# Cluster marks of a masked attention made in lots of four heads, most of them amid the attention loop

## The chip, the core and the metric

The kernel runs on one core of a Trainium2 chip. A core has five engines that run side by side, each through its own instructions in order: PE (TensorE, matrix products), DVE (VectorE), ACT (ScalarE), POOL (GpSimd) and SP, which here only issues transfers. They signal one another through semaphores. The metric is the device time of one execution in microseconds, taken as the median of several.

## What is computed

Two batches of eight heads with 768 tokens of 64 values go through an attention in which a query sees only keys of its own cluster. The result goes through two feed-forward layers.

```
q_assign = argmax(einsum('bhsd,hcd->bhsc', q_n, c_n))      # 16 centroids for each head
k_assign = argmax(einsum('bhsd,hcd->bhsc', k_n, c_n))
mask = q_assign[..., :, None] == k_assign[..., None, :]
scores = where(mask, scale * q @ k.T, -1e9)
attn_out = softmax(scores) @ v                             # 2 x 8 heads x 768 x 64
x = attn_out as (1536, 512)
h = x @ moe_w_in;   x = (h * sigmoid(1.702 h)) @ moe_w_out      # inner width 2048
h = x @ moe2_w_in;  x = layernorm(h * softmax(h)) * g @ moe2_w_out   # inner width 1024
```

## The kernel before, in words

**Marks of clusters.** A query's cluster becomes a column of 16 rows with a 0 in the row of its cluster and 1 elsewhere, a key's a column with -2^100 in its row and 0 elsewhere. They are appended to q and k as rows 64 to 79 (`q_high`, `k_low`), so the product of scores adds the mask by itself. The marks are made in eight lots. In the kernel before, a lot is one of q or k, one batch (eight heads) and half of the tokens (384). Its steps: `load_pairs` (SP, four head pairs of 64+64 rows, 768 KB), `sims_of` (PE, four products with the centroids into 4 x 32 rows of a PSUM bank), `copy_sims` (ACT, to `sims_t`), `tokens_of` (PE, three transposes, L465), `compare` (DVE, L919 and L921: a maximum for each token and head, and where it is reached), `rank_lot` (POOL, L1244, for the first of equals), `choose` (DVE, L930 and L935), `hots_of` (PE, transposes back, L476, for two lots at once) and `store_clusters` (ACT, L715, to `hot_t`; the second batch, and later reads of the first, go through `mask_rows` in HBM). All eight `compare`s and six of eight `choose`s stand ahead of the attention loop, the rest in its first steps.

**Attention.** It runs over 8 iterations (`it`) of two heads each; an iteration has 12 steps (`n`), and a step handles 128 queries against 768 keys. Numbers are split into a high and a low part for accuracy (`k_high`, `k_low`, and so on). In one step:

- PE: `turn` (L519, six transposes of the probabilities of the step six before), `scores_of` (L502 and L506, four products), and a third of `head_half` (L534): the product with v of half a head (three steps), 12 matmuls cut by `HEAD_SPLIT`. In steps n with n mod 3 = 0 stand the first 3, with n mod 3 = 1 the next 5, and with n mod 3 = 2 the last 4. The last 4 stand ahead of the step's scores, the others behind them.
- DVE: `row_max` (L959), sums and inverses for two steps at once (L967, L973), `x_sum` (L986, every third step, frees the bank `head_out` for the next half head), `turned_low` (L979, twice).
- ACT: `turned_high` (L772, twice), `exps` (L761), every third step `x_of_low_v` (L778), and `kq_high` (L728) once for each head.
- POOL: `scale_q`, `kq_low` (L1158, the low part of a head's q and k), the scaling of the probabilities by their sums (L1221), splits of v.
- SP: `place_head` moves the parts of a head (64 rows to other 64 rows, L328), waits for them, and then places its 16 rows of marks (L336).

PE runs one step ahead of the others. Transposes use a ring of three PSUM banks (`pt_bank`). Iteration 0 is written out, the others are a loop (`Fori`) on every engine, in which semaphores are compared with registers.

**Behind the attention** follow the first layer (three blocks; its weights come in `gelu_turn` and are split by POOL) and the second layer. The second layer's weights are loaded 512 KB at a time by `load_ln`, once in each iteration.

## Time and profile before

| | us |
|---|---|
| time before, median of 3 runs | 671.55 (671.33 to 674.67) |
| the profiled execution | 672.1 |
| span in its trace | 670.3 |

The profile shows, for each engine, when each instruction ran and for what the engine had waited. A line of the timeline gives start, duration, engine, source line, operation, what it writes and reads, the shape, and how many like it were merged; in square brackets stand the idle time ahead of it and what ended it. The chain of waits goes back from the last instruction, at each step to what released it. Attention's first scores start at 31.5 us and its last step is over at about 250 us. The first layer runs to about 530 us.

### The profile page before, as it was taken

What the parts mean: (1) busy time and instruction counts of PE and PEld (TensorE: products, weight loads), DVE (VectorE), ACT (ScalarE), POOL (GpSimd) and SP (SyncE); (2) the same over time, 40 slices, a digit from 0 to 9 for tenths busy, and PEclk for the clock granted to TensorE, in tenths of its full rate; (3) what the DMA queues carried; (4) which work ended last, traced back from release to release, by engine and by line L of the source; (5) the groups of instructions that cost most, each with busy time, mean ns of one, the idle gap of its engine ahead of it and who ended that gap; (6) DMA issues with size and microseconds to landing.
All of it is one profiled execution on the core that took longest, in us unless ns stands there. A gap on an engine that the chain in (4) does not pass through costs nothing.

```text
span 670.3 us, 11572 instructions
## 1 busy us (share of the span) xinstructions
PE 639.0 (95%) x3281; PEld 537.8 (80%) x3281; DVE 434.5 (65%) x759; ACT 321.0 (48%) x641; POOL 419.7 (63%) x590
## 2 busy tenths in 40 slices
PE   5689999999999999999999999999999999999998
PEld 1369989898989888788877888788888878888886
DVE  3779999999999985666657667562222554545352
ACT  1279999999999984222232222132222243324232
POOL 2677788798888886888878888878886100000000
PEclk9779999999999999999999999999999999999999
DMA  8866544544544421232222222222231022112101
GB/s 284 245 185 154 159 120 112 143 122 126 143 112 137 130 92 64 72 113 87 104 94 93 90 99 94 94 95 94 94 106 51 29 82 77 52 60 78 63 16 47
DMA packets 39601, 70.52 MB, mean 105 GB/s; under 512 B 4256, under 2 KB 22688, under 8 KB 39584
## 3 DMA queue, kind: packets, MB, share of 16 engines
q1 hardware_dynamic: 37568, 66.38, 33.1%
q10 hardware_dynamic: 2016, 3.93, 1.6%
q8 instruction: 8, 0.13, 0.1%
q14 instruction: 9, 0.07, 0.0%
HBM read 46.60 MB, written 4.72 MB: 77 GB/s over the span
## 4 chain that ended last, share of the span: by engine, by line
PE 68%; ACT 10%; issue 9%; DVE 5%; DMA 4%; POOL 2%; DVEq 1%; SPq 1%; ACTq 0%; POOLq 0%
PE banks L534 6%; PE banks L549 6%; PE banks L551 6%; PE banks L550 6%; PE banks L564 6%; PE banks L566 6%; PE banks L565 5%; PE banks L639 5%; ACT probs L761 4%; PE banks L519 4%; PE banks L672 3%; PE banks L671 3%; PE banks L670 3%; ACT probs_th L772 3%; PE banks L642 2%
## 5 line engine op out<-in xcount | busy, mean ns | idle before, releaser
L979 DVE TENSOR_TENSOR probs_tl<-banks,probs_th 128x384 fp32r<-128x384 f32 x192 | 100.5, 547 | 11.7 <-ACT probs_th L772 9.4
L959 DVE TENSOR_REDUCE neg_max<-banks 128x1 f32<-128x768 f32 x96 | 91.3, 951 | 8.6 <-PE banks L506 6.6
L772 ACT CAST probs_th<-banks 128x384 fp32r<-128x384 f32 x192 | 83.0, 485 | 20.8 <-PE banks L519 19.5
L761 ACT ACTIVATE probs<-banks,neg_max 128x768 f32<-128x768 f32 x96 | 88.3, 920 | 7.1 <-DVE neg_max L959 7.0
L953 DVE TENSOR_TENSOR gl<-gate,gh 128x512 fp32r<-128x512 f32 x48 | 48.2, 1003 | 66.8 <-ACT gh L746 66.8
L1145 POOL TENSOR_TENSOR wait_scrap<-half_power 128x1 f32<-128x1 f32 x176 | 46.4, 264 | 67.1 <-PE banks L566 33.7
L1221 POOL TENSOR_SCALAR probs<-probs,row_inv 128x768 f32<-128x768 f32 x96 | 87.0, 907 | 0.0
L1284 POOL TENSOR_TENSOR stat<-stat,half_power 128x1 f32<-128x1 f32 x12 | 6.6, 549 | 127.5 <-DVE stat L1092 127.5
L519 PE MATMUL banks<-ident,probs 128*128 128x128 f32 x576 | 79.0, 273 | 1.3 <-ACT hot_t L715 1.3
L534 PE MATMUL banks<-probs_th,v_parts 128*128 128x384 f32 x192 | 70.4, 367 | 9.8 <-DVE x_sums L986 9.8
L746 ACT CAST gh<-gate 128x512 fp32r<-128x512 f32 x48 | 29.8, 621 | 101.1 <-PE banks L566 52.7
L549 PE MATMUL banks<-xh,uph 128*128 (+1 forms) x192 | 76.0, 396 | 0.4 <-POOL upl L1194 0.4
L564 PE MATMUL banks<-gh,downh 128*128 128x512 f32 x192 | 75.8, 395 | 0.2
L566 PE MATMUL banks<-gh,downl 128*128 128x512 f32 x192 | 75.3, 392 | 0.0
L551 PE MATMUL banks<-xh,upl 128*128 (+1 forms) x192 | 75.3, 392 | 0.0
L550 PE MATMUL banks<-xl,uph 128*128 (+1 forms) x192 | 75.1, 391 | 0.0
L565 PE MATMUL banks<-gl,downh 128*128 128x512 f32 x192 | 74.8, 390 | 0.0
L1204 POOL TENSOR_TENSOR downl<-gelu_raw,downh 128x512 fp32r<-128x512 f32 x48 | 71.4, 1488 | 4.0
L519 PEld LDWEIGHTS banks<-ident,probs 128*128 128x128 f32 x576 | 68.5, 140 | 5.7 <-ACT hot_t L715 1.6
L742 ACT ACTIVATE gate<-banks 128x512 f32<-128x512 f32 x48 | 28.7, 599 | 81.8 <-PE banks L551 57.0
L1194 POOL TENSOR_TENSOR upl<-gelu_raw,uph 128x512 fp32r<-128x512 f32 x48 | 62.7, 1306 | 4.0
L534 PE MATMUL banks<-probs_tl,v_parts 128*128 128x384 f32 x192 | 65.1, 339 | 0.0
(100 smaller groups left out, 1346.1 us busy)
## 6 DMA issues: line engine op xcount, KB each, us to landing
gelu_raw<-w_gelu SPq DMA_DIRECT2D x48, 512.0 KB, 3.3
ln_raw<-w_ln SPq DMA_DIRECT2D x8, 512.0 KB, 4.3
pair_t<-q_t SPq DMA_DIRECT2D x4, 768.0 KB, 7.3
pair_t<-k_t SPq DMA_DIRECT2D x4, 768.0 KB, 8.2
kq_raw<-k_t SPq DMA_DIRECT2D x16, 192.0 KB, 3.5
kq_raw<-q_t SPq DMA_DIRECT2D x16, 192.0 KB, 3.7
q_parts<-k_high SPq DMA_DIRECT2D x16, 192.0 KB, 2.6
q_high<-k_high SPq DMA_DIRECT2D x16, 192.0 KB, 3.0
```

What stands on the lines that cost most here:

```text
L519: last = nc.tensor.transpose(pt_bank(n, c)[:, t * P:(t + 1) * P], probs[:, n % NP, k * P:(k + 1) * P], ident[:])
L534: last = nc.tensor.matmul(head_out, v_parts[j][:, i // 2].rearrange("p two d -> p (two d)"), part[half % 2][:, i // 2, :], start=i == 0, s ...
L549: nc.tensor.matmul(hidden[u], uph[u][:, cols], xh[:, k, tok], start=k == 0, stop=False)
L550: nc.tensor.matmul(hidden[u], uph[u][:, cols], xl[:, k, tok], start=False, stop=False)
L551: last = nc.tensor.matmul(hidden[u], upl[u][:, cols], xh[:, k, tok], start=False, stop=k == KT - 1)
L564: nc.tensor.matmul(acc[d], downh[u][:, cols], gh[u][:], start=first, stop=False)
L565: nc.tensor.matmul(acc[d], downh[u][:, cols], gl[u][:], start=False, stop=False)
L566: last = nc.tensor.matmul(acc[d], downl[u][:, cols], gh[u][:], start=False, stop=end)
L761: nc.scalar.activation(probs[:, n % NP, :].rearrange("p (c t) -> p c t", c=2), scores[n % 2], ACT.Exp, bias=neg_max[:, n % NP:n % NP + 1], ...
L772: nc.scalar.copy(probs_th[half % 2][:, c * CH:(c + 1) * CH, i * P:(i + 1) * P], pt_bank(n, c).rearrange("p (t s) -> p t s", t=CH)).then_in ...
L959: nc.vector.tensor_reduce(out=neg_max[:, col], in_=scores[n % 2], op=ALU.max, axis=mybir.AxisListType.XY, negate=True).then_inc(max_done, 1)
L979: nc.vector.tensor_tensor(probs_tl[half % 2][at], pt_bank(n, c).rearrange("p (t s) -> p t s", t=CH), probs_th[half % 2][at].bitcast(F32), ...
```

## The change

- A lot is now q **and** k of four heads (a quad) for half of the tokens, eight rows of 16 each side by side: rows 0 to 63 of `hot_t` are the marks for q, rows 64 to 127 those for k, and the factor of `store_clusters` is a vector (`mask_scale`). So lots 0 and 1 serve iterations 0 and 1, lots 2 and 3 iterations 2 and 3, and so on. `choose` writes its tile in two halves, one for q and one for k.
- Only lots 0 and 1 stand ahead of attention. Lot e of the others starts in step 1 (even e) or 7 (odd e) of iteration 0, 2 or 4: `sims_of` and `copy_sims` in that step, `rank_lot` one step on in POOL's order, `tokens_of` and `compare` two steps on, `choose` five, `hots_of` and `store_clusters` seven.
- The lots share the ring of three banks with the transposes: `unit_of` numbers all uses in PE's order, and `take_bank` waits until the use three before is over.
- `mask_rows` is gone: `place_head` copies the marks from `hot_t` by a transfer within SBUF. SP loads quad 0, the q and k of heads 0 and 1, places head 0, and then loads quad 1.
- `HEAD_SPLIT` becomes (0, 4, 8, 12), and all three thirds stand behind the scores of their step.
- The loop over iterations is written out on all engines, with constants in the waits.
- `load_ln` is called four times in each of the last two iterations.

```diff
...
-        KQ_STEP, STORE_STEPS, HOT_STEPS, CHOOSE_STEPS = 0, (2, 4), (3, 5), (0, 1)
+        KQ_STEP = 0
+        EARLY_LOTS = 2
+        LOT_STARTS = (1, 7)
+        SIMS_AT, RANK_AT, CHOOSE_AT, HOT_AT = 2, 1, 5, 7
+        def lot_start(e):
+            return (e // 2 - 1) * 2 * STEPS + LOT_STARTS[e % 2]
+        def lots_at(it, n, offset):
+            return [e for e in range(EARLY_LOTS, LOTS) if lot_start(e) + offset == it * STEPS + n]
+        unit_of = {}
+        for what in ("sims_t", "sims", "hot"):
+            for e in range(EARLY_LOTS):
+                unit_of[what, e] = len(unit_of)
+        for g in range(ITS * STEPS + TURN_LAG + AHEAD):
+            if g >= TURN_LAG + AHEAD:
+                for c in range(2):
+                    unit_of["turn", g - TURN_LAG - AHEAD, c] = len(unit_of)
+            for what, offset in (("sims_t", 0), ("sims", SIMS_AT), ("hot", HOT_AT)):
+                for e in lots_at(0, g, offset):
+                    unit_of[what, e] = len(unit_of)
...
+        def bank_free(unit):
+            if unit < TURN_BANKS:
+                return []
+            what, *which = unit_names[unit - TURN_BANKS]
+            if what == "turn":
+                return [(pt_low_done, 2 * which[0] + which[1] + 1)]
+            return [({"sims_t": sims_t_copied, "sims": compared, "hot": hot_t_done}[what], which[0] + 1)]
...
-                b, x, c = e // 4, e // 2 % 2, e % 2
-                if b > 0:
-                    sp.wait_ge(sims_t_done, e - 3)
-                half = slice(c * HALF, (c + 1) * HALF)
-                sp.dma_start(pair_t[x][:, :, half], (q_pairs, k_pairs)[x][b][:, :, half]
-                             ).then_inc(pair_loaded[x][c], 16)
+            def load_pairs(quad):
+                b, at = quad // 2, slice(quad % 2 * 2, quad % 2 * 2 + 2)
+                if quad >= 2:
+                    sp.wait_ge(sims_t_done, (quad - 1) * 2)
+                for c in range(2):
+                    half = slice(c * HALF, (c + 1) * HALF)
+                    for x in range(2):
+                        sp.dma_start(pair_t[x][:, at, half], (q_pairs, k_pairs)[x][b][:, at, half]
+                                     ).then_inc(pair_loaded[c], 16)
...
-                    src = mask_heads[x, bass.ds(h, 1)].rearrange("o c s -> (o c) s")
-                    if isinstance(it, int) and it == 0 and j == 0:
-                        sp.wait_ge(hot_t_done, x + 1)
-                        src = hot_t[x][0:C, :]
-                    sp.dma_start(dst.bitcast(F32), src).then_inc(qk_ready[j], 16)
+                    at = x * QUAD * C + h % QUAD * C
+                    sp.dma_start(dst.bitcast(F32), hot_t[h // QUAD % 2][at:at + C, :]).then_inc(qk_ready[j], 16)
...
-            for e in range(4):
-                load_pairs(e)
-            load_kq(0, 0)
-            for e in range(4, LOTS - 1):
-                load_pairs(e)
-            load_kq(0, 1)
+            load_pairs(0)
+            sp.dma_start(gains_sb[:], gains).then_inc(gains_loaded, 16)
+            for j in range(2):
+                load_kq(0, j)
             place_head(0, 0)
-            for x in range(2):
-                sp.wait_ge(hot_t_done, x + 1)
-                sp.dma_start(mask_rows[x, 0], hot_t[x][:]).then_inc(mask_stored[x], 16)
-            for j in range(2):
-                load_v(0, j)
+            load_pairs(1)
+            load_v(0, 0)
             load_kq(1, 0)
-            for x in range(2):
-                sp.wait_ge(mask_stored[x], 16)
             place_head(0, 1)
...
+            for it in range(1, ITS):
                 load_kq(it, 1)
                 place_head(it, 0)
                 load_v(it, 0)
-                if not last:
+                if it < ITS - 1:
...
+                if it % 2 == 1 and it // 2 + 2 < NQUAD:
+                    load_pairs(it // 2 + 2)
+                if it >= ITS - 2:
+                    sp.wait_ge(sims_done, LOTS)
+                    for part in range((it - ITS + 2) * ITS // 2, (it - ITS + 3) * ITS // 2):
+                        load_ln(part)
+            for j in range(2):
+                sp.wait_ge(qk_ready[j], 48 * ITS)
...
             def sims_of(e):
-                b, x, c = e // 4, e // 2 % 2, e % 2
-                pe.wait_ge(pair_loaded[x][c], (b + 1) * 16)
-                if e >= 4:
-                    pe.wait_ge(sims_t_copied, e - 3)
-                for n in range(HP):
-                    last = nc.tensor.matmul(sims_t_ps[x][n * 2 * C:(n + 1) * 2 * C, c, :], c_diag[:, n, :],
-                                            pair_t[x][:, n, c * HALF:(c + 1) * HALF], start=True, stop=True)
+                quad, c = e // 2, e % 2
+                pe.wait_ge(pair_loaded[c], (quad + 1) * 32)
+                dst = take_bank("sims_t", e)
+                for n in range(4):
+                    x, pair = n // 2, quad % 2 * 2 + n % 2
+                    last = nc.tensor.matmul(dst[n * 2 * C:(n + 1) * 2 * C, :], c_diag[:, pair, :],
+                                            pair_t[x][:, pair, c * HALF:(c + 1) * HALF], start=True, stop=True)
                 last.then_inc(sims_t_done, 1)
...
-                x, c = e // 2 % 2, e % 2
                 pe.wait_ge(sims_t_copied, e + 1)
-                if e >= 2:
-                    pe.wait_ge(compared, e - 1)
+                dst = take_bank("sims", e)
                 for i in range(CH):
-                    t = c * CH + i
-                    last = nc.tensor.transpose(sims[c][:, i * P:(i + 1) * P], sims_t[x][:, t * P:(t + 1) * P],
+                    last = nc.tensor.transpose(dst[:, i * P:(i + 1) * P], sims_t[e % 2][:, i * P:(i + 1) * P], ident[:])
+                last.then_inc(sims_done, 1)
...
+            def hots_of(e):
+                pe.wait_ge(hot_done, (e + 1) * 2)
+                dst = take_bank("hot", e)
+                for i in range(CH):
+                    last = nc.tensor.transpose(dst[:, i * P:(i + 1) * P], hot[e % RANKS][:, i * P:(i + 1) * P],
                                                ident[:])
-                last.then_inc(sims_done, 1)
...
-            for e in range(4):
-                sims_of(e)
-                if e >= 1:
-                    tokens_of(e - 1)
-            for e in range(4, LOTS):
-                tokens_of(e - 1)
-                sims_of(e)
-                if e < 6:
-                    hots_of(e - 4)
-            tokens_of(LOTS - 1)
+            for of in (sims_of, tokens_of, hots_of):
+                for e in range(EARLY_LOTS):
+                    of(e)
...
-                    if exists(it, n, 2 - c, STEPS):
-                        pe.wait_ge(pt_low_done, 2 * g - 2 + c)
+                    dst = take_bank("turn", g, c)
...
-            HEAD_SPLIT = (0, 3, 8, 12)
+            HEAD_SPLIT = (0, 4, 8, 12)
...
             def attention_turn(it, steps=STEPS, drain=False):
                 for n in range(steps):
-                    first = isinstance(it, int) and it == 0
-                    if first and n in HOT_STEPS:
-                        hots_of(2 + HOT_STEPS.index(n))
-                    if first and n == TURN_LAG + AHEAD:
-                        pe.wait_ge(hot_t_done, LOTS // 2)
                     if exists(it, n, TURN_LAG + AHEAD, STEPS) and not (drain and n >= TURN_LAG + AHEAD):
                         turn(*lagged(it, n, TURN_LAG + AHEAD, STEPS))
-                    for c, lag in enumerate(HEAD_LAG + AHEAD + c for c in range(3)):
-                        if c in (2,) and exists(it, n, lag, STEPS) and (n - lag) % CH == CH - 1 and not (
-                                drain and n >= lag):
-                            head_half(*lagged(it, n, lag, STEPS), c)
                     if not drain:
                         scores_of(it, n)
                     for c, lag in enumerate(HEAD_LAG + AHEAD + c for c in range(3)):
-                        if c in (0, 1) and exists(it, n, lag, STEPS) and (n - lag) % CH == CH - 1 and not (
+                        if exists(it, n, lag, STEPS) and (n - lag) % CH == CH - 1 and not (
                                 drain and n >= lag):
                             head_half(*lagged(it, n, lag, STEPS), c)
+                    for of, offset in ((sims_of, 0), (tokens_of, SIMS_AT), (hots_of, HOT_AT)):
+                        for e in lots_at(it, n, offset):
+                            of(e)
...
+                if e >= 2:
+                    act.wait_ge(sims_done, e - 1)
+                nc.scalar.copy(sims_t[e % 2][:], turn_bank(unit_of["sims_t", e])).then_inc(sims_t_copied, 1)
+            def store_clusters(e):
+                quad, c = e // 2, e % 2
+                act.wait_ge(hot_ps_done, e + 1)
+                if e == 0:
+                    act.wait_ge(mask_scale_set, 2)
+                if quad >= 2:
+                    for j in range(2):
+                        act.wait_ge(qk_ready[j], 48 * 2 * (quad - 1))
+                nc.scalar.activation(hot_t[quad % 2][:, c * HALF:(c + 1) * HALF], turn_bank(unit_of["hot", e]), ACT.Copy,
+                                     scale=mask_scale[:]).then_inc(hot_t_done, 1)
...
-                if g >= 2:
-                    dve.wait_ge(hot_ps_done, g - 1)
-                nc.vector.tensor_tensor(heads(hot[x][:, c * HALF:(c + 1) * HALF]), ranks,
-                                        most[:].unsqueeze(2).to_broadcast([P, G, C]),
-                                        ALU.is_equal if x else ALU.not_equal).then_inc(hot_done, 1)
-            for b in range(B):
-                for e in range(4 + CHOICE_LAG):
-                    if e < 4:
-                        compare(b * 4 + e)
-                    if e >= CHOICE_LAG and b * 4 + e - CHOICE_LAG < LOTS - len(CHOOSE_STEPS):
-                        choose(b * 4 + e - CHOICE_LAG)
+                if e >= RANKS:
+                    dve.wait_ge(hot_ps_done, e - RANKS + 1)
+                for x in range(2):
+                    def side(ap):
+                        return ap.rearrange("p (i x h c) -> p i x h c", i=CH, x=2, c=C)[:, :, x]
+                    most = rank_max[r][:].rearrange("p (i x h) -> p i x h", i=CH, x=2)[:, :, x]
+                    nc.vector.tensor_tensor(side(hot[r][:]), side(rank[r][:]),
+                                            most.unsqueeze(3).to_broadcast([P, CH, QUAD, C]),
+                                            ALU.is_equal if x else ALU.not_equal).then_inc(hot_done, 1)
...
-            for e in range(LOTS):
+            scale_q(0, 0)
+            for e in range(EARLY_LOTS):
                 rank_lot(e)
-                if e == 2:
-                    scale_q(0, 0)
-                if e == 3:
-                    for c in range(2):
-                        kq_low(0, 0, c)
-                if e == 4:
-                    scale_q(0, 1)
+            for c in range(2):
+                kq_low(0, 0, c)
+            scale_q(0, 1)
             for c in range(2):
...
```

PE ahead of attention. `pair_t` holds q and k as loaded, `sims_t` the copied products, `hot` the marks by token. In the kernel before, the eight rows before the first scores, and the scores:

```order
L465 MATMUL banks<-ident,sims_t 128x128 x3
L453 MATMUL banks<-pair_t,c_diag 32x384 x4
L476 MATMUL banks<-ident,hot 128x128 x6
L465 MATMUL banks<-ident,sims_t 128x128 x3
L453 MATMUL banks<-pair_t,c_diag 32x384 x4
L465 MATMUL banks<-ident,sims_t 128x128 x3
L453 MATMUL banks<-pair_t,c_diag 32x384 x4
L465 MATMUL banks<-ident,sims_t 128x128 x3
L502 MATMUL banks<-k_high,q_parts 128x384 x2
```

In the changed kernel, from the products of both early lots on:

```order
L481 MATMUL banks<-pair_t,c_diag 32x384 x8
L489 MATMUL banks<-ident,sims_t 128x128 x6
L497 MATMUL banks<-ident,hot 128x128 x6
L516 MATMUL banks<-k_high,q_parts 128x384 x2
L520 MATMUL banks<-k_low,q_high 128x384 x2
L516 MATMUL banks<-k_high,q_parts 128x384 x2
L520 MATMUL banks<-k_low,q_high 128x384 x2
L481 MATMUL banks<-pair_t,c_diag 32x384 x4
```

Two lots are left ahead of the scores, and the third one's products (last row) follow behind the scores of step 1.

PE within attention, a step with n mod 3 = 2 (`probs_th`, `probs_tl` are the turned probabilities of a half head). Before:

```order
L512 REGISTER_ALU
L516 ISA
L519 MATMUL banks<-ident,probs 128x128 x3
L516 REGISTER_ALU
L519 MATMUL banks<-ident,probs 128x128 x3
L534 MATMUL banks<-probs_th1,v_parts0 128x384
L534 MATMUL banks<-probs_tl1,v_parts0 128x384
L534 MATMUL banks<-probs_th1,v_parts0 128x384
L534 MATMUL banks<-probs_tl1,v_parts0 128x384
L498 REGISTER_ALU
L502 MATMUL banks<-k_high0,q_parts0 128x384 x2
L506 MATMUL banks<-k_low0,q_high0 128x384 x2
```

Changed, the same step of iteration 2, which also holds the products of no lot:

```order
L531 MATMUL banks<-ident,probs 128x128 x6
L516 MATMUL banks<-k_high0,q_parts0 128x384 x2
L520 MATMUL banks<-k_low0,q_high0 128x384 x2
L546 MATMUL banks<-probs_th1,v_parts0 128x384
L546 MATMUL banks<-probs_tl1,v_parts0 128x384
L546 MATMUL banks<-probs_th1,v_parts0 128x384
L546 MATMUL banks<-probs_tl1,v_parts0 128x384
```

The scores stand ahead of the last third of the half head, and the register instructions are gone.

DVE within attention, steps 2 and 3. Before (loop body):

```order
L959 TENSOR_REDUCE neg_max<-banks 128x1
L967 TENSOR_REDUCE row_sum_e<-row_sum 128x2
L984 ISA
L986 ISA x2
L986 TENSOR_TENSOR x_sums<-banks,x_sums 64x384
L977 ISA
L979 TENSOR_TENSOR probs_tl1<-banks,probs_th1 128x3x128
L973 RECIPROCAL row_inv<-row_sum_e 128x2
```

Changed, iteration 2, steps 5 and 6, where the choice of lot 4 stands:

```order
L994 TENSOR_TENSOR x_sums<-banks,x_sums 64x384
L986 TENSOR_TENSOR probs_tl0<-banks,probs_th0 128x3x128 x2
L966 TENSOR_REDUCE neg_max<-banks 128x1
L974 TENSOR_REDUCE row_sum_e<-row_sum 128x2
L986 TENSOR_TENSOR probs_tl0<-banks,probs_th0 128x3x128
L980 RECIPROCAL row_inv<-row_sum_e 128x2
L986 TENSOR_TENSOR probs_tl0<-banks,probs_th0 128x3x128
L933 TENSOR_REDUCE rank_max0<-rank0 128x24
L944 TENSOR_TENSOR hot0<-rank0,rank_max0 128x3x64 x2
L966 TENSOR_REDUCE neg_max<-banks 128x1
```

Three instructions of the lot stand between the low parts of step 6 and the row maxima of step 7; the register instructions between row maxima and `x_sums` are gone.

## Rows read from the trace of the kernel before

**Rows 1.** Timeline: PE ahead of attention (start us, duration us, engine, line)
```profile
9.75 0.90 PE L465 MATMUL banks<-ident,sims_t 128*128 128x128 f32 x3
```
**Rows 2.** Timeline: POOL ahead of attention
```profile
20.26 2.59 POOL L1158 TENSOR_TENSOR k_low<-kq_raw,k_high 128x384 fp32r<-128x384 f32 x2
```
**Rows 3.** Chain of waits, 20 to 60 us (start us, us, what)
```profile
22.87 5.32 DMA q_parts<-k_low
...
28.83 2.62 DMA k_low<-hot_t
...
43.08 0.71 ACT hot_t L715
43.81 4.06 DMA mask_rows<-hot_t
```
**Rows 4.** The page's transfers (count, size, median us to landing)
```profile
q_parts<-k_low SPq DMA_DIRECT2D x16, 192.0 KB, 2.7
```
**Rows 5.** Timeline: DVE, row maxima of iteration 0, steps 0, 5, 6, 7, 8
```profile
33.26 0.96 DVE L959 TENSOR_REDUCE neg_max<-banks 128x1 f32<-128x768 f32 x1 [1.37 <-PE banks L506]
...
42.58 0.96 DVE L959 TENSOR_REDUCE neg_max<-banks 128x1 f32<-128x768 f32 x1 [0.26 <-PE banks L506]
...
46.73 0.96 DVE L959 TENSOR_REDUCE neg_max<-banks 128x1 f32<-128x768 f32 x1 [0.77 <-PE banks L506]
...
48.65 0.95 DVE L959 TENSOR_REDUCE neg_max<-banks 128x1 f32<-128x768 f32 x1
...
50.44 0.95 DVE L959 TENSOR_REDUCE neg_max<-banks 128x1 f32<-128x768 f32 x1
```
**Rows 6.** Windows: stretch us, busy us of PE, PEld, DVE, ACT, POOL, PEclk, DMA share, GB/s
```profile
36.00:40.00 4.00, 4.00 (x15) 3.48 (x15) 2.99 (x7) 2.62 (x5) 3.61 (x6) 0.50 0.64 140
...
72.50:126.50 54.00, 51.25 (x337) 47.85 (x335) 50.57 (x105) 49.73 (x113) 45.53 (x68) 1.00 0.49 129
```
**Rows 7.** Waits, 72 to 234 us (in total, times, longest)
```profile
PE banks L534 <- DVE x_sums L986: 8.0, 25, 0.6
```
**Rows 8.** Timeline: one turn of three steps in iteration 4, all engines
```profile
136.79 0.92 ACT L761 ACTIVATE probs<-banks,neg_max 128x768 f32<-128x768 f32 x1
...
137.22 0.51 PE L506 MATMUL banks<-k_low,q_high 80*128 80x384 f32 x2
...
137.77 0.96 DVE L959 TENSOR_REDUCE neg_max<-banks 128x1 f32<-128x768 f32 x1
137.83 0.48 ACT L778 COPY x_sums<-banks 64x384 f32 x1
...
138.85 0.55 DVE L986 TENSOR_TENSOR x_sums<-banks,x_sums 64x384 f32 x1
...
139.46 0.45 PE L534 MATMUL banks<-probs_th,v_parts 128*128 128x384 f32 x1 [0.37 <-DVE x_sums L986]
```
**Rows 9.** Timeline: DVE in iteration 0, step 11, which has constants in its waits
```profile
56.51 0.96 DVE L959 TENSOR_REDUCE neg_max<-banks 128x1 f32<-128x768 f32 x1
57.38 0.54 DVE L986 TENSOR_TENSOR x_sums<-banks,x_sums 64x384 f32<-64x384 f32 x1
```
**Rows 10.** Timeline: the parts of a lot ahead of attention
```profile
24.35 0.85 PE L453 MATMUL banks<-pair_t,c_diag 128*32 128x384 f32 x8
24.46 0.56 DVE L919 TENSOR_REDUCE sims_max<-banks 128x24 f32<-128x384 f32 x1 [1.41 <-PE banks L465]
25.05 0.56 DVE L921 TENSOR_TENSOR rank<-banks,sims_max 128x384 f32<-128x384 f32 x1
...
25.53 0.54 DVE L930 TENSOR_REDUCE rank_max<-rank 128x24 f32<-128x384 f32 x1
25.70 1.00 POOL L1244 TENSOR_TENSOR rank<-rank,first_rank 128x384 f32<-128x384 f32 x1 [0.54 <-DVE rank L921]
...
26.11 1.00 DVE L935 TENSOR_TENSOR hot<-rank,rank_max 128x384 f32<-128x384 f32 x1
...
34.71 0.56 DVE L935 TENSOR_TENSOR hot<-rank,rank_max 128x384 f32<-128x384 f32 x1
```

148 lines of the change are left out of this document (63 added, 85 removed).

## Prediction

> **What bounds the kernel now.** I read the shares of the windows first, then who waits for whom, then the timeline of one turn of the attention loop, and last the chain of waits at the start. The change touches only the time up to the end of attention, about 250 of 670 us; the two layers behind it keep their work and order. Within attention no engine stands out: in 54 us, two iterations, PE is busy for 51.25, DVE for 50.57, ACT for 49.73 and POOL for 45.53 [rows 6]. So the loop goes round a chain through several engines. The waits name its seam: PE waits for DVE's `x_sum`, 25 times in 162 us for 8.0 us, so 0.33 us in every turn of three steps (about 6.75 us) [rows 7]. The timeline shows the turn: `exps` on ACT from 136.79, the copy of the half head from 137.83, `x_sum` on DVE at 138.85, and at 139.46 PE starts the next half head, behind which stand the transposes that ACT waits for next [rows 8]. `x_sum` starts 0.54 us after the copy is over (138.31) since DVE's row maxima hold it up, and they had waited until 137.73 for scores that stand behind the last third of the half head. The next most tightly loaded part is DVE: where it has no waits, a step goes by in 1.79 us (48.65 to 50.44, step 7 of iteration 0 [rows 5]); with the sums (about 0.13 in every second step) and an `x_sum` (0.5 in every third), three steps need some 6.1 of the 6.75 us. That leaves 0.6 us a turn, and this is where the lots go.
>
> **First term, the start: -8.9 us.** Now the first scores start at 31.45, at the landing of head 0's marks (28.83 + 2.62) [rows 3]. What the change leaves ahead of them: the first lot's load has the size of the first transfer before (768 KB), the second's as well, so PE turns the first lot's tokens at 9.75 as before [rows 1]. A lot's comparison takes 0.56 + 0.56 and two gaps of 0.03, so 1.2 us [rows 10]: over at 11.9 for lot 0 and 13.1 for lot 1, as the tokens of lot 1 follow at once, without a further lot's products between. POOL's ranking (1.00 [rows 10]) of lot 1 is over at 14.1, and then `kq_low` follows with 2.59 [rows 2], until 16.7; before, it was over at 22.85. The marks (choice, transposes, `store_clusters`) are ready at about 17.5, before they are asked for. The move of the low parts took 5.32 us here [rows 3] amid five other loads; the median of its 16 is 2.7 [rows 4]. Ahead of it now only head 1's 192 KB pieces are under way, so I take 2.8, with 5.3 as the other end: landed at 19.6. From there to the first scores it was 3.3 us before (28.19 to 31.45) [rows 3], and the transfers are the same. First scores at 22.6 instead of 31.5: -8.9, between -6.4 and -9.3.
>
> **Second term, the filling of the loop: -2.2 us.** In iteration 0 the row maxima of step 6 follow those of step 5 after 4.15 us (42.58 to 46.73), the next after 1.92 [rows 5]. In that gap ACT writes `hot_t` until 43.79 and `mask_rows` goes to HBM until 47.87 [rows 3]; PE waits for both. The change has neither at this place: -2.2. The clock stays as it was: it stood at 0.50, 1.2 GHz, from 36 to 40 us, nine microseconds into dense work, and at 1.00 later [rows 6], and I expect the same number of slow steps. Lot 2's products and tokens (twice 0.85 and 0.55 at the low clock) and its comparison fall into steps 1 to 3, where there are no transposes and half heads yet, and PE waits for `exps` of two steps ago: nothing. Head 1 must be placed until step 6, 13 us after the start; SP comes to it behind head 0, four loads of pairs, v and two more, some 5 us, then needs about 9 us as before (`kq_high` to landed marks). This is close; its bound is +2 us.
>
> **Third term, the turn of the loop: -7.2 us.** With the scores ahead of the last third, the row maxima before `x_sum` start when DVE is free, 0.1 us earlier in one kind of turn and 0.2 in the other. The constants in the waits take away two register instructions between them: in iteration 0, which has constants, `x_sum` starts 0.87 us after the row maxima [rows 9], in the loop 1.08 after (137.77 to 138.85) [rows 8]. In the turn shown this is 0.28, in the other kind 0.20, on average 0.24 us. It is less than PE's 0.33 of waiting, so PE doesn't take it back, and `HEAD_SPLIT` moves one matmul from the second to the first third, with the same sum ahead of the transposes. 30 turns by 0.24: -7.2. The bounds are -9.9 (all of PE's waiting) and 0, if ACT's copy now waits for the last third: by my count of PE's instructions that is over within 0.1 us of when ACT comes to it.
>
> **Fourth term, six lots amid attention: +15.2 us.** PE: 0.85 (products at the full clock) and twice 0.3 (transposes: 0.55 with the last one's run-out) [rows 10]. The products stand between the second third and the transposes that ACT waits for, so they count in full, 0.8. DVE: the comparison, 1.2 at the end of step 3 or 9; ahead of the next row maxima there is a slack of 0.4 (in the turn shown, ACT's `exps` start 0.4 us after their maxima), so it costs 0.8. The choice: a maximum of 0.54 and two halves of a tile that took 1.00 with POOL at work and 0.56 without (25.70 and 26.11 against 34.71) [rows 10]. The slow one ended at 27.11, 0.41 us after POOL's instruction (25.70 + 1.00). So I take it that a piece can't run beside POOL's reading of the same memory, and ends some 0.2 us behind POOL's current instruction, most of which take 0.9 to 1.0. The first half catches the rest of one of them, the second half a whole one: 0.55 + 0.35 + 1.1 = 2.0 us, less 0.4 of slack: 1.6. The ends are 0.7 (two halves of 0.28 and the maximum, less the slack) and 2.4. Marks turned back and stored fall where PE and ACT have 0.3 to 0.5 us to spare: nothing. The products of an odd lot stand one step behind an even lot's choice, in whose delay they disappear. So a pair of lots costs 0.8 + 0.8 + 1.6 + 0.8 + 1.6 = 5.6 us, and the first pair, whose first two items lie in the filling, 4.0: 15.2 in all. PE's work alone, 1.45 each, would give 8.7.
>
> The Trainium skill (SBUF — State Buffer, SBUF: two separate sides) states such a lock: a DVE instruction with two SBUF inputs and a GpSimd one exclude each other for a whole instruction. Without it, two halves at half of 1.00 would make the choice 1.55 us and this term about 12.5; the ends 0.41 us behind POOL's agree with the lock.
>
> **Nothing** for the rest: POOL has 8 of 54 us to spare for a ranking of 1.00; SP has fewer transfers; weights of the first layer start behind four more loads of 512 KB, some 5 us later, of which POOL's waits in the last iteration cover most (bound +1.5).
>
> **Sum.** 672.1 - 8.9 - 2.2 - 7.2 + 15.2 = 669.0 for an execution like the profiled one, which lies 0.55 above the median of the runs: 668.4.
>
> **The rivals.** (1) The lots vanish in the idle time of DVE and PE, down to PE's own 8.7: 662. For it speaks that a delay of DVE lets PE run ahead; against it, that the turn has 0.6 us of slack and a lot brings over 3 us. (2) Slower: DVE becomes the bound at the lots. If both halves of the choice wait for a whole instruction of POOL (2.8 us), and the ring of three banks, which a lot's use makes one narrower, lets PE wait for the low parts of the step just before, nothing of a lot is hidden: 1.2 + 2.8 on DVE and no slack, 4 us each, 24 in all: 677. It decides from 3.6 us a lot, where the sum passes 675. For it speaks DVE's load; against it, that iterations 1, 3, 5 to 7 are nearly free of lots. (3) The third term fails, as ACT waits for the half head: 675.5 by the sum. (4) The change doesn't start attention as early as it says, since head 0's moves or head 1's placement stay at their slow ends: 4 us less, 672.5.
>
> **Chances.** My sum 0.42, rival (1) 0.20, (2) 0.12, (3) 0.11, (4) 0.15. The range leaves out the far end of (2) and mixtures beyond (1): 661.5 to 676. A measurement of this kernel tells 0.5%, 3.4 us, from no change. Faster by more: all of (1) and half of my own case, whose middle lies 3.15 below: 0.42. Slower by more: (2) and two thirds of (3), 0.19. Within: the rest, 0.39.
>
> **What would show it.** In the trace of the changed kernel: first scores at 22.6 (right within 1 us); the row maxima of steps 5 to 7 of iteration 0 about 2 us apart; iterations 6 and 7, which have no lots, 26.0 instead of 27.0 us, with PE's waits for `x_sum` down to 0.1 a turn and `x_sum` 0.87 behind the row maxima; iterations 2 and 4 longer than those by about 4, and 3 and 5 by 1.6; halves of `hot` of about 0.35 and 1.1 us. A wrong third term shows as idle time of ACT ahead of the copy of the half head; a wrong fourth as waits of PE's transposes for low parts, or as lots without any trace in the cadence.

## The result, and the profile after

| | before | after |
|---|---|---|
| median, us (range, runs) | 673.11 (671.33 to 676.15, 4) | 693.34 (692.08 to 695.46, 4) |
| span of the profiled execution, us | 670.3 | 691.4 |

The ratio is 1.031 (95% interval 1.028 to 1.034): 3% slower, where 668.4 us and a range up to 676 were forecast.

A row maximum on DVE begins every step, so the distances of their starts are a ruler for attention. Iteration lengths (row maxima of step 0 to the next step 0), with two of the experiments (1 and 3) beside them:

| us | first row maxima | it 0 | 1 | 2 | 3 | 4 | 5 | 6 |
|---|---|---|---|---|---|---|---|---|
| before | 33.26 | 25.51 | 27.46 | 26.99 | 27.04 | 27.01 | 27.01 | 27.00 |
| after | 24.45 | 32.17 | 29.18 | 35.45 | 28.36 | 35.45 | 28.32 | 28.09 |
| without lots 2 to 7 | 23.71 | 24.56 | 26.21 | 26.18 | 26.20 | 26.21 | 26.23 | 29.52 |
| lots 12 steps apart | 25.70 | 27.89 | 32.39 | 32.39 | 32.39 | 32.38 | 32.39 | 26.65 |

Attention starts 8.8 us earlier, and a turn of the loop is shorter. Iterations 2 and 4 hold a whole even lot and the products and comparison of the odd one; they take 35.45 us instead of 27. Iterations 3 and 5 hold the odd lot's choice and marks and take 28.3. So a pair of lots adds 11.4 us to the 52.4 of two iterations without lots.

The chain of waits of the changed kernel at the start (answers [rows 3]; start us, us, what):

```profile
17.12 2.73 DMA q_parts<-k_low
...
20.48 2.16 DMA k_low<-hot_t
...
22.68 1.01 PE banks L516 x2
```

The low parts move in 2.73 us (5.32 before) and the first scores start at 22.68 us instead of 31.50.

The filling (answers [rows 5]): the timeline of DVE, row maxima of steps 5 and 6 of iteration 0, then PE's scores of step 6 and SP's moves of head 1:

```profile
33.90 0.94 DVE L966 TENSOR_REDUCE neg_max<-banks 128x1 f32<-128x768 f32 x1
38.73 0.96 DVE L966 TENSOR_REDUCE neg_max<-banks 128x1 f32<-128x768 f32 x1 [2.56 <-PE banks L520]
```

```profile
37.05 1.01 PE L516 MATMUL banks<-k_high,q_parts 128*128 128x384 f32 x2 [2.55 <-DMA k_low<-hot_t]
```

```profile
27.71 0.60 SPq L365 DMA_DIRECT2D q_high<-k_high  x1
29.22 0.46 SPq L365 DMA_DIRECT2D q_parts<-k_low  x1
33.27 0.46 SPq L365 DMA_DIRECT2D k_high<-k_high  x1
```

The step from 5 to 6 is 4.83 us, longer than the 4.15 that were to become 1.95: PE waits 2.55 us for head 1's marks. SP could issue `k_high`'s move at 33.27 only, since the move issued at 27.71 took 5.54 us to land. The loads of the second quad had been issued ahead of it; no run takes them away, so that they are the reason is argued.

PE's waits in the same gap of the kernel before (timeline of PE, iteration 0):

```profile
43.83 0.87 PE L519 MATMUL banks<-ident,probs 128*128 128x128 f32 x6 [1.29 <-ACT hot_t L715]
...
45.71 0.62 PE L502 MATMUL banks<-k_high,q_parts 128*128 128x384 f32 x2 [1.01 <-DMA k_low<-mask_rows]
```

There PE waited 1.29 us for ACT's marks and 1.01 us for the landing of head 1's rows of marks. It did not wait for the transfer to `mask_rows` until 47.87 [rows 3], as the row maxima of step 6 start at 46.73.

One turn of three steps in iteration 6, which has no lots (answers [rows 8]; timeline, ACT, DVE and PE):

```profile
197.84 0.95 DVE L966 TENSOR_REDUCE neg_max<-banks 128x1 f32<-128x768 f32 x1
...
198.11 0.47 ACT L780 COPY x_sums<-banks 64x384 f32<-64x384 f32 x1
...
198.82 0.56 DVE L994 TENSOR_TENSOR x_sums<-banks,x_sums 64x384 f32<-64x384 f32 x1
...
199.53 0.41 PE L546 MATMUL banks<-probs_th,v_parts 128*128 128x384 f32 x1
```

From the row maxima to `x_sum` it is 0.98 us (1.08 before, [rows 8]), and PE's half head has no wait ahead of it. Over the four turns of an iteration the distance is 0.86 to 1.04 us, 0.95 on average, against 1.02 before; the row maxima themselves start 0.27 us ahead of ACT's copy of the half head instead of 0.06. The windows of two iterations without lots, in the changed kernel without lots 2 to 7 (answers [rows 6]; stretch, us, busy us of PE, PEld, DVE, ACT, POOL, clock, DMA share, GB/s):

```profile
74.48:126.86 52.38, 51.29 (x338) 48.16 (x337) 50.22 (x105) 49.54 (x113) 45.76 (x69) 1.00 0.46 114
```

The same work as before, 1.6 us shorter, and PE busy for 98% of it.

Now the lots. The waits of PE in attention, 20 to 270 us (answers [rows 7]; in total, times, longest):

```profile
PE banks L516 <- DMA k_low<-hot_t: 9.0, 3, 4.2
PE banks L497 <- ACT sims_t L708: 7.0, 3, 2.4
PE banks L531 <- DVE rank L925: 5.2, 5, 1.1
PE banks L531 <- ACT sims_t L708: 2.4, 2, 1.2
PE banks L531 <- DVE probs_tl L986: 2.2, 3, 0.9
PE banks L489 <- ACT hot_t L720: 2.0, 3, 0.7
PE banks L546 <- DVE x_sums L994: 1.9, 7, 0.3
```

`x_sum`'s 8.0 us are down to 1.9. The first row is no wait on lots: it is the start, head 1 (2.55 us) and head 14 (2.29 us). The rows with `sims_t`, `rank` and `hot_t` are 16.6 us of new waits on lots. Iteration 2, the parts of lot 4 (PE products at L481, ACT's copy at L708, a turn at L531, comparison at L923 and L925, choice at L933 and L944):

```profile
88.00 0.85 PE L481 MATMUL banks<-pair_t,c_diag 128*32 128x384 f32 x8
...
91.65 0.48 ACT L708 COPY sims_t<-banks 128x384 f32<-128x384 f32 x1
...
92.27 0.85 PE L531 MATMUL banks<-ident,probs 128*128 128x128 f32 x6 [1.21 <-ACT sims_t L708]
...
96.66 0.55 DVE L923 TENSOR_REDUCE sims_max<-banks 128x24 f32<-128x384 f32 x1
...
97.24 0.56 DVE L925 TENSOR_TENSOR rank<-banks,sims_max 128x384 f32<-128x384 f32 x1
...
97.95 0.85 PE L531 MATMUL banks<-ident,probs 128*128 128x128 f32 x6 [1.05 <-DVE rank L925]
...
104.67 0.54 DVE L933 TENSOR_REDUCE rank_max<-rank 128x24 f32<-128x384 f32 x1
...
104.80 0.93 POOL L1235 TENSOR_SCALAR probs<-probs,row_inv 128x768 f32<-128x768 f32 x1
105.25 1.76 DVE L944 TENSOR_TENSOR hot<-rank,rank_max 128x192 f32<-128x192 f32 x2
...
105.66 1.14 POOL L1166 TENSOR_TENSOR k_low<-kq_raw,k_high 128x384 fp32r<-128x384 f32 x1
```

The products were over at 88.85, but ACT copied them at 91.65, since its copy stands at the end of a step, behind the exponentials; two steps on, the transposes that need the bank wait 1.21 us for it. The choice takes 0.54 + 1.76 = 2.3 us. The run with lots 12 steps apart shows one lot by itself. Its step lengths against those without a lot:

| step | what of the lot | without, us | with, us | more, us |
|---|---|---|---|---|
| 1 | products on PE | 1.80 | 2.63 | 0.83 |
| 2 | the turn waits for ACT's copy of them | 2.38 | 3.52 | 1.14 |
| 3 | tokens; comparison on DVE | 1.98 | 3.38 | 1.40 |
| 4 | | 2.12 | 2.30 | 0.18 |
| 6 | choice on DVE | 2.14 | 4.40 | 2.26 |
| 7 | | 2.00 | 1.80 | -0.20 |
| 9 | marks turned and stored | 1.87 | 2.44 | 0.57 |

These are 6.2 us for a lot by itself, all of it visible in the cadence. In the changed kernel a pair costs 11.4 and not 12.4: the odd lot's products in step 7 lengthen nothing (1.79 us against 1.80 with the even lot alone), as was forecast, and its choice costs 1.44 us (step 0 of iteration 3, 3.84 against 2.40).

Last, the layer norm's loads. SP in iterations 6 and 7 (timeline; then one row of the chain of waits, 222 to 245 us), and PE's scores of head 14 behind them:

```profile
222.40 1.98 SPq L388 DMA_DIRECT2D ln_raw<-w_ln  x4
...
230.51 0.46 SPq L365 DMA_DIRECT2D q_parts<-k_low  x1
236.94 0.46 SPq L365 DMA_DIRECT2D k_high<-k_high  x1
```

```profile
227.87 9.05 DMA q_high<-k_high
```

```profile
240.47 0.62 PE L516 MATMUL banks<-k_high,q_parts 128*128 128x384 f32 x2 [2.29 <-DMA k_low<-hot_t]
...
242.33 1.48 PE L531 MATMUL banks<-ident,probs 128*128 128x128 f32 x6
```

```profile
240.00:244.00 4.00, 3.54 (x16) 3.44 (x17) 1.30 (x3) 1.22 (x3) 1.98 (x3) 0.69 0.63 145
```

Behind four loads of 512 KB the move of head 14 issued at 227.87 lands after 9.05 us (the median of its 16 is 3.0), and SP issues `k_high`'s move 6.4 us after the one before it. PE waits 2.29 us. Its granted clock is then 0.69 on average over the four microseconds shown (0.50, 1.2 GHz, from 242 to 244 us), and six transposes take 1.48 us instead of 0.82.

### The profile page after: what moved, and what is told of

The parts are those of the page before. It is cut to its first block, busy times and chain, and to the rows that moved or that the text cites. A ratio compares the mean times of both kernels' runs of the same rounds, so it can differ in the third digit from the quotient of the medians.

```text
span 691.4 us, 10571 instructions
## 1 busy us (share of the span) xinstructions
PE 638.9 (92%) x3281; PEld 537.4 (78%) x3281; DVE 437.0 (63%) x769; ACT 322.0 (47%) x645; POOL 420.3 (61%) x590
## 4 chain that ended last, share of the span: by engine, by line
PE 63%; ACT 10%; DMA 8%; DVE 7%; issue 6%; POOL 5%; SPq 1%; DVEq 0%; POOLq 0%; ACTq 0%
PE banks L561 6%; PE banks L563 6%; PE banks L562 6%; PE banks L576 5%; PE banks L578 5%; PE banks L577 5%; PE banks L643 5%; PE banks L531 4%; PE banks L546 4%; ACT probs L762 4%; ACT probs_th L773 3%; PE banks L676 3%; PE banks L675 3%; PE banks L674 3%; PE banks L646 2%
## 5 line engine op out<-in xcount | busy, mean ns | idle before, releaser
L531 PE MATMUL banks<-ident,probs 128*128 128x128 f32 x576 | 80.8, 277 | 11.4 <-DVE rank L925 5.2
L531 PEld LDWEIGHTS banks<-ident,probs 128*128 128x128 f32 x576 | 68.1, 142 | 21.2 <-issue 12.2
L546 PE MATMUL banks<-probs_th,v_parts 128*128 128x384 f32 x192 | 67.4, 351 | 4.0 <-DVE x_sums L994 1.9
L516 PE MATMUL banks<-k_high,q_parts 128*128 128x384 f32 x192 | 59.5, 392 | 10.0 <-DMA k_low<-hot_t 9.0
```

What stands on the lines that cost most here:

```text
L531: last = nc.tensor.transpose(dst[:, t * P:(t + 1) * P], probs[:, n % NP, k * P:(k + 1) * P], ident[:])
L546: last = nc.tensor.matmul(head_out, v_parts[j][:, i // 2].rearrange("p two d -> p (two d)"), part[half % 2][:, i // 2, :], start=i == 0, s ...
```

## The experiments

Theory A: the lots cost more than they were priced at. Theory B: the start or the turn has failed and the lots are cheap. Within A three causes stood against each other: DVE's amount of work, the ring of three banks that a lot's use makes narrower, and order and locks at single places. Ratios are against the kernel before on the same chip.

### 1. Without lots 2 to 7 (`no_lots`)

```diff
-            return [e for e in range(EARLY_LOTS, LOTS) if lot_start(e) + offset == it * STEPS + n]
+            return []
-        LOTS = 2 * NQUAD
+        LOTS = 2
```

> The changed kernel without lots 2 to 7: their loads (but quad 1's), products, comparisons, rankings, choices, transposes and stores are left out, and all heads get the marks of quad 0. It measures what the six lots cost amid attention. Both theories: iterations 2 to 5 fall to 26.2 us each, the cadence that iteration 6 of the changed kernel shows, so 2 x 9.2 + 2 x 2.1 = 22.6 us less there, some 6 us less in iterations 0 and 1, and a time near 665. If iterations 2 to 5 stay over 27, the loop written out costs something by itself.

Measured: 660.34 us, ratio 0.982 (0.979 to 0.985); iterations of 26.2 us. So the lots cost 33 us, more than twice the 15.2 of the fourth term, and B falls. What is left is still 7 us above the 653.2 that the other terms give: iterations 6 and 7 are 3.3 and 1.6 us longer than in experiment 11, where the layer norm's loads are spread, and the filling is 1.2 and the turn some 1.2 us short of their terms.

### 2. Little work on DVE for these lots (`light`)

```diff
-                nc.vector.tensor_reduce(out=sims_max[r][:], in_=sim, op=ALU.max, axis=AX_X).then_inc(sims_max_done, 1)
+                nc.vector.tensor_reduce(out=sims_max[r][:, some], in_=sim[:, some], op=ALU.max, axis=AX_X).then_inc(sims_max_done, 1)
...
+                    if e >= EARLY_LOTS:
+                        nc.vector.tensor_tensor(side(hot[r][:])[:, 0, 0], side(rank[r][:])[:, 0, 0],
+                                                most[:, 0, 0:1].to_broadcast([P, C]),
+                                                ALU.is_equal if x else ALU.not_equal).then_inc(hot_done, 1)
+                        continue
```

(`some` is the first of 24 groups.)

> The changed kernel with DVE's work for lots 2 to 7 cut to one group of 16 columns of 24 (comparison, maximum and both halves of the choice: some 0.15 to 0.2 us each instead of 3.9 in all); PE, ACT, POOL and all waits stay. The marks of quads 1 to 3 are thus mostly left out. Theory of the ring (a lot's use of the three transpose banks ties PE to ACT's and DVE's current step, so that it loses its lead of one step): half or more of the 11.4 us a pair of lots stays, iterations 2 and 4 at 30 to 31 us. Rival, the work on DVE: iterations 2 and 4 fall to about 28 (26.2 and twice PE's 0.8), and PE's waits in the ring vanish with it.

Measured: 683.80 us, 1.017 (1.014 to 1.020). Nearly all of DVE's elements are gone, and 9.5 us with them; 23.5 are left. I read that at first as a proof against DVE and for the ring. It was neither, as experiments 4 and 8 show: step 6 still took 4.11 us, since the two tiny halves of the choice took 1.85.

### 3. Lots 12 steps apart (`apart`)

```diff
-        LOT_STARTS = (1, 7)
+        LOT_STARTS = (1, 13)
```

> The changed kernel with LOT_STARTS (1, 13) instead of (1, 7): the odd lot starts a whole iteration after the even one, with the same work. Then three uses ahead of the even lot's marks in the ring no longer stands the odd lot's product tile, on which PE waits 2.4 us for ACT's copy, nor the marks three ahead of the odd lot's tokens (0.7 us). Theory of the ring: 3 us less for each pair, 9 in all, a time of 684. Rival, the work on DVE: a lot more in one iteration and one less in the other, no change of the sum, 692 to 694.

Measured: 692.99 us, 1.031 (1.027 to 1.034), no change. The longest of the waits (2.4 us of a lot's marks for the next lot's copied products) is gone, and every lot costs 6.2 us by itself. A wait's length in the list was no price: others took its place.

### 4. Empty places in the ring (`empty_units`)

Experiment 1, but each lot's three places in the ring stay, unused:

```diff
-        LOTS = 2 * NQUAD
+        LOTS = 2
...
+        def lots_at(it, n, offset):
+            return []
...
-                for e in lots_at(0, g, offset):
+                for e in skipped_at(0, g, offset):
                     unit_of[what, e] = len(unit_of)
...
+            if what != "turn" and which[0] >= EARLY_LOTS:
+                return bank_free(unit - TURN_BANKS)
```

> The kernel without lots 2 to 7 (660.3 us), but every lot still takes its three places in the ring of three banks (products, tokens, hots; 18 places in all) and leaves them empty. No engine has work of these lots. So the time over 660.3 is the price of the narrower ring alone: after an empty place the second half of the next step's transposes must wait for the low parts of the step just before, and not of the one before that. With DVE's work of the lots nearly gone the time was 683.8, so PE's and ACT's work, the ring and the order share 23.5 us. PE's products and transposes are 1.45 us a lot, 8.7 in all. My theory, that most of the rest is the ring: 0.5 us a place, 669 us (666 to 673), with iterations 2 and 4 longest. Rival, the work itself in PE's and ACT's order is what costs, and a skipped bank by itself costs nothing: 660 to 662 us, all iterations at 26.2.

Measured: 662.44 us, 0.983 (0.979 to 0.987), and every iteration from 1 to 5 is 26.20 or 26.21 us. The windows of iterations 2 and 3, with the six empty places of a pair of lots:

```profile
77.24:129.65 52.41, 51.40 (x338) 48.12 (x337) 50.24 (x105) 49.61 (x113) 45.73 (x69) 1.00 0.47 114
```

The ring, the theory that I held after experiment 2, costs nothing in the loop by itself. (By the medians it is 2 us over experiment 1, but the traced execution, 659.59 us, is not longer than that of experiment 1, 660.57: iteration 0 is 2.05 us longer, where PE waits 2.3 us instead of 1.4 for head 1's marks, and iteration 6 is 2.2 shorter.) What costs is that a place is held until somebody has done its work.

### 5. The lots' pieces ahead of scores and exponentials (`copy_first`)

```diff
+                    for of, offset in ((sims_of, 0), (tokens_of, SIMS_AT), (hots_of, HOT_AT)):
+                        for e in lots_at(it, n, offset):
+                            of(e)
                     if not drain:
                         scores_of(it, n)
```

(PE; on ACT `copy_sims` and `store_clusters` go ahead of `exps` in the same way.)

> The changed kernel with the lots' pieces earlier within their step: on PE the products, tokens and hots go ahead of the scores instead of behind the half head's third, on ACT the copies of products and marks go ahead of the exponentials. Theory that the waits of PE's transposes for ACT's copy (1.2 us each, two in iterations 2 and 3) and for the marks' copy are what costs: they go, at about 1 us a lot, 687 us. Rival, by what the run with lots 12 steps apart showed: a delay around the ring only changes its name, since scores and row maxima now come 0.8 us later and DVE, with its comparison behind, has no slack: 690 to 697 us, with the waits of the copy gone and waits for DVE's low parts or comparison in their place.

Measured: 687.89 us, 1.019 (1.015 to 1.024): 5.4 us less by the medians, 7.7 by the ratios, each of which is known to 2 or 3 us. The theory had said 6. Step 2 is 0.33 us longer than without a lot instead of 1.14, iterations 2 and 3 are 33.8 and 27.7. A pair is 2.3 us cheaper, so the place of the pieces, on PE and ACT together, was about 1 us a lot. The rest stays.

### 6. The choice in one instruction (`one_choice`)

```diff
-                    nc.vector.tensor_tensor(side(hot[r][:]), side(rank[r][:]),
-                                            most.unsqueeze(3).to_broadcast([P, CH, QUAD, C]),
-                                            ALU.is_equal if x else ALU.not_equal).then_inc(hot_done, 1)
+                nc.vector.tensor_tensor(heads(hot[r][:]), heads(rank[r][:]),
+                                        rank_max[r][:].unsqueeze(2).to_broadcast([P, G, C]), ALU.is_equal
+                                        ).then_inc(hot_done, 2)
...
-                                     scale=mask_scale[:]).then_inc(hot_t_done, 1)
+                                     bias=mask_bias[:], scale=mask_scale[:]).then_inc(hot_t_done, 1)
```

> The changed kernel with the choice's two halves in one instruction (equal for q and k alike; the store of the marks turns q's side over by its scale and a bias). Same elements, one meeting with POOL's lock in the place of two: 1.76 + 0.54 us of choice should become about 1.0 + 0.54, the step that holds it 3.6 instead of 4.41 us, and the time 6 times 0.8 less: 688 us (686.5 to 690). Rival: DVE's wait at this place isn't the lock but the amount of work, and the number of instructions is indifferent: 693 us.

Measured: 687.72 us, 1.023 (1.020 to 1.026), 5 to 6 us less. Step 6 is 3.52 us instead of 4.41, with the same elements. (In iteration 2 the single instruction took 0.82 us, the two halves 1.76.) That the time came out as forecast is in part luck: 6 times 0.8 had been counted, but only the even lots gain. Iteration 2 is 0.8 us shorter and iteration 3 the same (28.32 against 28.36 us); of the rest in the trace, 2.55 us lie in iteration 0, where none was expected. Experiment 8 shows why the odd lots gain nothing.

### 7. One input in place of two (`light_one_input`)

Experiment 2 with another kind of tiny instruction:

```diff
-                        nc.vector.tensor_tensor(side(hot[r][:])[:, 0, 0], side(rank[r][:])[:, 0, 0],
-                                                most[:, 0, 0:1].to_broadcast([P, C]),
-                                                ALU.is_equal if x else ALU.not_equal).then_inc(hot_done, 1)
+                        nc.vector.tensor_scalar(side(hot[r][:])[:, 0, 0], side(rank[r][:])[:, 0, 0], 1.0, None,
+                                                ALU.mult).then_inc(hot_done, 1)
```

> The run with little work on DVE (683.8 us; of lots 2 to 7 one head in twelve times two is compared and chosen, and marked), and in addition each of the two small pieces that write the marks reads one tile of memory times 1.0 instead of comparing two tiles. In the 683.8 us run these two pieces of 16 columns still took 1.85 us, beside POOL's instructions, and the step that holds them was 4.11 us long where one without a lot takes 2.14. If that is the lock of DVE against POOL, and it needs two inputs in memory, the pieces fall to 0.2 us, the step to about 2.5 and the time by 6 times 1.5: 675 us (673 to 677). Rival: the pieces wait for something else that stands there (POOL's ranking, the transposes that read the tile), or one input is locked as well: 683.8 us.

Measured: 685.73 us, 1.021 (1.017 to 1.024); step 6 is 4.09 us, the pieces 1.85. My condition, two inputs, was wrong. It left open whether it is a lock at all.

### 8. A reduction in their place (`light_reduce`)

```diff
-                        nc.vector.tensor_tensor(side(hot[r][:])[:, 0, 0], side(rank[r][:])[:, 0, 0],
-                                                most[:, 0, 0:1].to_broadcast([P, C]),
-                                                ALU.is_equal if x else ALU.not_equal).then_inc(hot_done, 1)
+                        nc.vector.tensor_reduce(out=side(hot[r][:])[:, 0, 0, 0:1], in_=side(rank[r][:])[:, 0, 0],
+                                                op=ALU.max, axis=AX_X).then_inc(hot_done, 1)
```

> The run with little work on DVE (683.8 us), its two pieces at the place of the choice made a third kind of instruction: a tensor_reduce of 16 columns of the ranks into one column of the same tile (the marks are not chosen by it). If the 1.85 us are a lock against GpSimd that only some kinds of instruction meet, the pieces take 0.16 us each like the reduce ahead of them, the step falls from 4.11 to about 2.5 us (2.14 without a lot) and the time by 6 times 1.6: 674 us (672 to 677). If the wait belongs to the place or to the tile that is written, the step stays at 4.1 and the time at 684.

Measured: 679.42 us, 1.006 (1.004 to 1.009). By the ratios that is 7 us less than experiment 2 (by the medians 4.4; the kernel before was 2.4 us slower in this measurement), where 10 were expected. The trace is of an execution of 687.05 us, longer than the median; against the trace of experiment 2 it starts 1.3 us later and its iterations 0 and 6 are 3.2 and 2.9 us longer. The steps used here lie in iteration 2 at a clock of 1.00. The instructions themselves decide the question. First the timeline of DVE and POOL in experiment 2:

```profile
99.86 0.90 POOL L1243 TENSOR_SCALAR probs<-probs,row_inv 128x768 f32<-128x768 f32 x1
99.91 1.85 DVE L948 TENSOR_TENSOR hot<-rank,rank_max 128x16 f32<-128x16 f32 x2
100.73 1.00 POOL L1174 TENSOR_TENSOR k_low<-kq_raw,k_high 128x384 fp32r<-128x384 f32 x1
```

then the tiles `hot`, `rank_max` and `rank` in it (line, engine, operation, count: shortest/median/longest ns, first and last start):

```profile
L948 DVE TENSOR_TENSOR hot<-rank,rank_max x2: 874/962/1051, 99.9 to 100.7; 128x16 f32<-128x16 f32 x2
L936 DVE TENSOR_REDUCE rank_max<-rank x1: 160/160/160, 99.7 to 99.7; 128x1 f32<-128x16 f32 x1
L927 DVE TENSOR_TENSOR rank<-banks,sims_max x1: 174/174/174, 92.7 to 92.7; 128x16 f32<-128x16 f32 x1
```

the tile `hot` with one input:

```profile
L948 DVE TENSOR_SCALAR hot<-rank x2: 875/971/1067, 100.2 to 101.0; 128x16 f32<-128x16 f32 x2
```

and with reductions:

```profile
L948 DVE TENSOR_REDUCE hot<-rank x4: 158/166/172, 102.8 to 120.0; 128x1 f32<-128x16 f32 x4
```

Sixteen columns take 0.16 us by a reduction and 0.17 by a comparison one of whose inputs is a bank, but 0.87 and 1.05 by a comparison of two tiles and 0.88 and 1.07 by a product of one tile. In experiment 2 the first piece ends at 99.91 + 0.87 = 100.78, with POOL's instruction (99.86 + 0.90 = 100.76); the second at 101.76, with POOL's next (100.73 + 1.00 = 101.73). Two instructions in a row each wait for a whole instruction of POOL, whatever they have to do. The odd lot of the same run gives the other half of the comparison (timeline, then the tile `hot`):

```profile
118.32 1.01 POOL L1174 TENSOR_TENSOR k_low<-kq_raw,k_high 128x384 fp32r<-128x384 f32 x1
...
118.55 0.90 DVE L948 TENSOR_TENSOR hot<-rank,rank_max 128x16 f32<-128x16 f32 x2
```

```profile
L948 DVE TENSOR_TENSOR hot<-rank,rank_max x2: 163/490/816, 118.5 to 119.3; 128x16 f32<-128x16 f32 x2
```

The first piece ends at 118.55 + 0.82 = 119.37, with POOL's instruction (119.33). The second, the same instruction, takes 0.16 us: POOL has only an instruction of one column then. That is a lock against POOL, and it depends on the kind of instruction, as the comparison with an input in a bank (at 92.68) and the reductions (at 102.82) ran beside large instructions of POOL in 0.16 to 0.17 us. The choice met it twice in the even lots and once in the odd ones; in the changed kernel the two halves take 1.76 us in an even lot and 0.93 in an odd one. With reductions step 6 is 2.50 us instead of 4.11, 1.6 us less. But steps 7 and 8 grow by 0.65 and 0.13 (the end of one lot meets the start of the next), and a pair of lots gets cheaper by 2.2 us (62.28 to 60.06) and not by 3.2.

The Trainium skill (SBUF — State Buffer, Who interferes with whom) names both conditions: two SBUF inputs, or a kind of instruction that can use both ports, among them `tensor_scalar`; `tensor_reduce` never contends on this chip. The rows above agree.

### 9. PE alone (`pe_only`)

Experiment 7, with ACT's copies of products and marks cut from 384 to 8 columns.

```diff
-                nc.scalar.copy(sims_t[e % 2][:], turn_bank(unit_of["sims_t", e]))
+                cut = HALF if e < EARLY_LOTS else 8
+                nc.scalar.copy(sims_t[e % 2][:, 0:cut], turn_bank(unit_of["sims_t", e])[:, 0:cut])
```

> As the run with one input on DVE, and ACT's copies of products and marks of lots 2 to 7 cut from 384 to 8 columns (heads 4 to 15 get their marks' rows from the first four). PE's products, tokens and hots are all there: 1.45 us a lot, 8.7 in all. If PE has no slack and the other engines' parts are gone, 660.3 + 8.7 = 669 us (667 to 671), and the turn behind the products no longer waits 1.2 us for the copy, so ACT's part was the 5 to 6 us between. Rival: ACT's copies lie in its idle time and PE's place and order cost it all: no change against the run with one input (675).

Measured: 681.75 us, 1.014 (1.011 to 1.017), 4 us under experiment 7, not 6, and 21 over experiment 1. It is not PE alone: the tiny choice still meets the lock (step 6 4.09 us), and the turn in step 2 still waits 0.9 us for a copy of 8 columns, since the copy's place is late and not its length. Amounts of work on ACT explain 4 us.

### 10. Both taken away (`reduce_copy_first`)

Experiments 5 and 8 together.

> The same with the lots' pieces ahead of the scores on PE and ahead of the exponentials on ACT. Left of a lot are then PE's 1.45 us (8.7 in all over the 660.3 us without lots, so 669) and what ACT's two copies of 0.5 us push back. If waits behind ACT's place were most of the rest: 669 to 671 us, 4 below light_reduce. If it is only the amount of PE's and ACT's work that counts, their place changes nothing: 674.

Measured: 680.72 us, 1.009 (1.006 to 1.012), the same as experiment 8. Iterations 2 and 3 take 32.66 and 26.96 us, against 32.78 and 27.28. Its steps say why: step 2 is 0.8 us shorter and step 7 is 1.2 longer. In 75 to 135 us PE waits now at the lots' own transposes:

```profile
PE banks L489 <- ACT hot_t L720: 1.4, 1, 1.4
PE banks L497 <- ACT sims_t L708: 1.1, 1, 1.1
```

Moved ahead of the scores, marks and tokens of one lot come before ACT has emptied the bank of the other, and hold the scores up. So 7.2 us a pair stay (32.66 + 26.96 - 2 × 26.2), of which PE's own work is 2.9. The 4.3 between are not taken apart further.

### 11. The layer norm's loads spread (`ln_spread`)

```diff
+            PARTS = {(ITS - 3, 1): (0, 1), (ITS - 2, 0): (2,), (ITS - 2, 1): (3, 4), (ITS - 1, 0): (5,), (ITS - 1, 1): (6, 7)}
```

(one or two parts behind each head's v, instead of four at once)

> The changed kernel with the eight loads of the second layer's weights spread behind five placements of heads (2, 1, 2, 1, 2) instead of four each in the last two iterations. Theory of the loads: the move of head 14's low parts no longer lands 6.4 us after its issue, PE's 2.3 us wait at the start of iteration 7 and the slow clock behind it go, and the start of the first layer's weights comes earlier: 3 to 5 us less. Rival: the placement was late for another reason, no change.

Measured: 689.91 us, 1.026 (1.023 to 1.029), 3.4 us less; iteration 6 is 26.21 us instead of 28.09, and iteration 7 is 1.9 us shorter. Iterations 0, 2 and 4, which the edit doesn't touch, differ by -1.4, +0.9 and +0.9 us between the two traces, so single iterations with lots are known to about a microsecond only.

### 12. Three changes together (`all_three`)

Experiments 5, 6 and 11.

> Three changes on top of the changed kernel: the pieces of lots ahead of scores and exponentials (alone -5.4 us), the layer norm's loads spread over the last iterations (alone -3.4), and the choice in one instruction (expected -5). If they lie at different places they add up: 679.5 us (677.5 to 682). If the choice in one gives nothing: 684.5.

Measured: 684.43 us, 1.017 (1.013 to 1.020): 8.9 us less than the changed kernel, near 5.4 + 3.4, what experiments 5 and 11 gave by their medians (by the ratios it is 9 against 11, within the intervals). The choice in one gives nothing on top: step 6 is 3.50 us instead of 4.39, step 7 is 2.65 instead of 1.79. Again a gain at one place is given back at the next.

### 13. The kernel before with one part of the loop change, or both

`b_order`, the sums' thirds all behind the scores (the lines that ran the last third ahead of them go as well):

```diff
-            HEAD_SPLIT = (0, 3, 8, 12)
+            HEAD_SPLIT = (0, 4, 8, 12)
...
-                        if c in (0, 1) and exists(it, n, lag, STEPS)
+                        if exists(it, n, lag, STEPS)
```

> The kernel before with only one part of the change: HEAD_SPLIT (0, 4, 8, 12), and the last third of a half head behind the scores; loops stay. By the prediction's third term the row maxima start 0.1 to 0.2 us earlier in each turn: 0.6 us an iteration, 4.5 us less, 667. Rival: the gain comes only with constants in the waits, no change.

Measured: 674.09 us, 1.000 (0.998 to 1.002), iterations of 27.24 us. The waits of 90 to 144 us, two iterations, have two rows that the kernel before has not:

```profile
DVE x_sums L982 <- ACT x_sums L774: 2.2, 4, 0.6
...
ACT x_sums L774 <- PE banks L534: 1.2, 4, 0.3
```

With the new order alone ACT's copy waits for the last third in two of four turns, and `x_sum` for the copy, which is what the prediction named as the case in which its third term is 0.

`b_unroll`, the loops written out on all engines:

```diff
-            attention_turn(0)
-            with pe.Fori(1, ITS) as it:
+            for it in range(ITS):
```

> The kernel before with only the loops of attention written out, with constants in the waits; the order stays. By the prediction's third term x_sum starts up to 0.2 us earlier in every second turn: 0.3 us an iteration, 2 to 3 us less, 669. Rival: the register instructions are hidden behind row maxima, no change; or fetching straight code costs time, slower.

Measured: 673.42 us, 0.998 (0.997 to 1.000), iterations of 27.0 us.

`b_both`:

> The kernel before with both, the order and the loops written out, but with all lots ahead of attention as before. The changed kernel's iteration 6 took 26.2 us instead of 27.0: 7 iterations by 0.8, so 5.5 to 6 us less than before, 666. If this is right, the third term of the prediction holds, and the 20 us are all due to the lots and the loads.

Measured: 666.29 us, 0.988 (0.985 to 0.991), iterations of 26.2 us. Neither part gives anything alone, both together give 7.9 us by the medians (5.7 between the two spans in the traces): the kernel before with the loop of the changed kernel and all lots ahead. The two waits of `b_order` are gone again. With `b_early_store` it is the fastest whole kernel here. Windows of two of its iterations:

```profile
87.93:140.40 52.47, 51.35 (x339) 48.23 (x337) 50.27 (x106) 49.64 (x114) 45.94 (x70) 1.00 0.52 134
```

`b_early_store`, the same with the second lot's store a step earlier:

```diff
-        KQ_STEP, STORE_STEPS, HOT_STEPS, CHOOSE_STEPS = 0, (2, 4), (3, 5), (0, 1)
+        KQ_STEP, STORE_STEPS, HOT_STEPS, CHOOSE_STEPS = 0, (2, 3), (3, 4), (0, 1)
```

> The kernel before with both parts of the loop change (sums' thirds behind the scores, loops written out: 666.3 us), and in iteration 0 the second lot's transposes and its store one step earlier, steps 4 and 3 instead of 5 and 4. In the 666.3 us kernel the scores of step 6 waited 1.96 us for the landing of the marks' rows, the clock then fell for 4 us, and iteration 0 took 29.2 us where the kernel before has 25.5. If the store is 0.9 us earlier the wait shrinks by as much and the clock may stay up: 663 to 665.5 us, iteration 0 of 26 to 28.3. Rival: the rows are late because of something else (both stores' transfers, or the choice before them): iteration 0 still 29, 666.3 us.

Measured: 666.25 us, 0.987 (0.983 to 0.991). The 29.2 us of the expectation were a misreading. One row of `b_both`'s timeline holds two row maxima, so thirteen steps had been counted:

```profile
38.77 1.94 DVE L953 TENSOR_REDUCE neg_max<-banks 128x1 f32<-128x768 f32 x2 [0.95 <-PE banks L506]
```

Its iteration 0 took 26.81 us. It fell to 25.54, but the first row maxima came at 34.08 instead of 32.49, behind a move of 6.43 us; the time did not change. Whether it is worth anything stays open.

## Why the prediction was wrong

**Start, -8.9: right.** 24.45 against 33.26, so -8.8; the scores at 22.68 where 22.6 was said, and the move of the low parts 2.73 us where 2.8 was taken. (The working gives 19.6 + 3.3 = 22.9 and not 22.6; the last part took 2.8 us and not 3.3.) Single traces scatter: with this start the first row maxima came between 23.26 and 25.75, 24.55 on average of 13 traces, with the old one between 31.74 and 34.69, 33.25 on average of 5.

**Filling, -2.2: failed.** Without lots iteration 0 gives 0.95 (25.51 to 24.56). Two steps failed. "PE waits for both": in the gap PE waited for ACT's marks and for the landing of head 1's rows, not for the transfer to `mask_rows`, and the landing stays in the changed kernel. And "this is close": head 1's marks land late, and PE waits 2.55 us at step 6. I had the bound and took the value without it.

**Turn, -7.2: right in size, not in its parts.** Iterations went from 27.0 to 26.2, 0.20 us in each of four turns, where 0.24 was worked out. The order was to give 0.1 to 0.2 us a turn and gave 0.21 (the row maxima's start against ACT's copy). The constants were to bring `x_sum` nearer to the row maxima by 0.21; they did so in one turn of four, the one shown in [rows 8] (1.08 to 0.87 in `b_unroll`), 0.07 on average. That the two misses cancel in part is luck. Experiment 13 adds that the two causes which I added up as independent don't add: each alone gives nothing. With the order alone ACT's copy comes late; why that wait goes when the loops are written out stays open.

**Lots, +15.2: failed, it is 33.** This is the step that decided. By parts, against one lot by itself in experiment 3: the products 0.8, measured 0.83. The comparison 0.8 because 0.4 of its 1.2 would lie in slack: 1.40. The choice 1.6, as 2.0 less the same slack: 2.26, with the next step giving 0.2 back; the instructions took 2.3 us, so the duration was close and the deduction wrong. The marks "nothing": 0.57. And a term that was not in the sum, 1.14 us, in which the turn waits for a bank that ACT empties at the end of its step. A pair was to cost 5.6 us and cost 11.4. Two mistakes in one: slack seen on DVE between two waits is not slack of the loop, when PE, DVE and ACT are each busy for 95 to 98% of it (51.3, 50.2 and 49.5 of 52.4 us); and of a moved step I priced what it does, but not how long it holds a shared bank.

**The lock** was seen in the right row (0.41 us behind POOL, [rows 10]) and priced nearly right: 1.45 us for the two halves, measured 1.76 in an even lot and 0.93 in an odd one. It is a part of the 33 us, not most of them: without it (experiment 8) a pair of the light lots was 2.2 us cheaper.

**Layer norm's loads, "nothing" with a bound of 1.5: failed.** 3.4 us by experiment 11, all of it ahead of the first layer: the last row maxima come 3.4 us earlier there. The loads held up head 14's moves, and PE's wait was followed by a lower clock.

**The rivals.** (2) had the sign and the right engine but stopped at 24 us and rested partly on the ring, which experiment 4 takes out. (1) was the opposite of what happened. (3)'s condition, ACT waiting for the half head, came true in `b_order` and not in the changed kernel. As a ledger against the kernel before: -8.8 start, -0.95 filling, -5.3 turn in iterations 1 to 6, +33.3 lots (iterations 0 to 5 against those without lots, the late head 1 among them), +3.4 loads: +21.7, measured 21.1 in the spans.

## What to carry to other kernels

Ahead of the loop a lot cost at most about 1.5 us (8.8 us for six, 2.6 of them a faster move of the low parts), inside it 5.6 on average and 6.2 by itself: an idle share of 2 to 5% on each engine is not room, and work moved into such a loop should be priced at its full length on each engine it visits, plus the time it holds a shared bank. Putting whoever empties such a bank ahead of the long work in its step gave 5.4 us (experiment 5), but nothing on top of experiment 8. Before splitting a DVE instruction that runs beside POOL, count instructions and not elements; each can wait for a whole instruction of POOL.

## What the runs showed of the hardware

- A DVE instruction of 16 columns took 0.16 us as a reduction and 0.82 to 1.07 us as a product or comparison in memory beside a large instruction of POOL, then ending with it; the same comparison took 0.16 us where POOL had one column to do; one of 128x384 took 0.82 us, two of half its size 1.76.
- Writing out the loops gave nothing measurable by itself (0.998, 0.997 to 1.000), yet 1.0 us an iteration (27.24 to 26.22) once the order of PE was changed.
- The same move of 192 KB took 9.05 us behind four loads of 512 KB, with a median of 3.0.
- A wait of PE of 2.29 us in dense work was followed by transposes at 1.48 instead of 0.82 us at a granted clock of 0.50 (242 to 244 us), one of 1.21 us (at 92.27) by transposes at 0.85.
